# The first layer job's clipped-square activation: last step moved from VectorE to GpSimd

## The reference, cut to what matters

```python
scores = q @ k.T / 8                       # 4 batches, 8 heads, 576 rows, 64 wide
attn   = softmax(scores where they are among the row's 32 largest)
x      = attn @ v                          # laid out as 2304 tokens x 512
h      = x @ w_in                          # layer 1, 2048 wide
g      = where(h >= 1, h, where(h <= -1, 0, (h + 1)**2 / 4))
x      = g @ w_out
h      = maximum(x @ w_in2, 0)             # layer 2
out    = (h * h) @ w_out2
```

## Time and profile before

| | |
|---|---|
| Median of 3 runs | 1271.18 us (1269.45 to 1271.53) |
| The profiled execution | 1268.48 us, its span 1266.7 us |
| PE busy in the span | 1189.1 us, 94% |
| DVE / ACT / POOL busy | 846.9 / 799.9 / 748.4 us |
| The stretch of job 0's activations on DVE | 127.7 to 219.8 us |

### The profile page before, as it was taken

The page is one execution under the profiler, slowest core; times in us unless marked ns, Lnnn a source line. Parts: engine busy times, 40 slices in busy tenths (PEclk is TensorE's granted clock), DMA queues, the critical chain, the costliest instruction groups (busy, mean ns, idle before and its releaser), DMA issues.

```text
span 1266.7 us, 24472 instructions
## 1 busy us (share of the span) xinstructions
PE 1189.1 (94%) x8760; PEld 1130.0 (89%) x8760; DVE 846.9 (67%) x1894; ACT 799.9 (63%) x1797; POOL 748.4 (59%) x620
## 2 busy tenths in 40 slices
PE   3777888999999999999999999999999999999998
PEld 2667888988889999999999999999999999999997
DVE  7898999899798799989899987878740111110000
ACT  6887666767666667676666766566654565654443
POOL 4778678777888676777857675755652222222222
PEclk9756999999999999999999999999999999999999
DMA  7798456675879953154348841456439400780000
GB/s 259 266 360 326 183 205 241 225 280 193 307 279 362 388 206 105 64 170 141 126 143 287 299 150 45 126 177 201 124 118 369 172 34 1 292 306 18 18 17 17
DMA packets 96264, 240.65 MB, mean 190 GB/s; under 512 B 7824, under 2 KB 47760, under 8 KB 83856
## 3 DMA queue, kind: packets, MB, share of 16 engines
q1 hardware_dynamic: 96144, 239.09, 52.9%
HBM read 167.23 MB, written 71.83 MB: 189 GB/s over the span
## 4 chain that ended last, share of the span: by engine, by line
PE 71%; ACT 9%; DVE 8%; POOL 5%; issue 3%; DMA 3%; SPq 0%; ACTq 0%; POOLq 0%
PE h_ps L600 21%; PE y_ps L621 15%; PE y_ps L615 11%; PE pv_ps L559 6%; PE score_ps L600 6%; DVE top L903 4%; PE tr_ps L532 4%; PE score_ps L497 3%; DVE rest L905 3%; ACT prob L718 2%; POOL s_sb L1085 2%; POOL prob L1090 1%; POOL kq_lo L1068 1%; ACT s_sb L695 1%; PE pv_ps L571 1%
## 5 line engine op out<-in xcount | busy, mean ns | idle before, releaser
L1103 POOL TENSOR_TENSOR g_lo<-g_sb,g_hi 128x256 fp32r<-128x256 f32 x288 | 217.5, 755 | 415.4 <-ACT g_hi L813 226.9
L600 PE MATMUL h_ps<-xt_hi,w_in 128*128 128x256 f32 x1880 | 391.0, 291 | 3.5 <-DVE xt_lo L951 1.7
L600 PEld LDWEIGHTS h_ps<-xt_hi,w_in 128*128 128x128 f32 x1880 | 309.3, 191 | 6.4 <-ACT r_sb L795 2.3
L903 DVE MAX8 top<-rest 128x8 f32<-128x576 f32 x432 | 304.4, 745 | 0.4
L600 PE MATMUL h_ps<-xt_lo,w_in 128*128 128x256 f32 x940 | 266.1, 283 | 0.0
L1085 POOL TENSOR_SCALAR s_sb<-s_sb,top 128x576 f32<-128x576 f32 x126 | 223.9, 1777 | 44.2 <-DVE top L903 44.1
L615 PE MATMUL y_ps<-g_hi,w_out 128*128 128x256 f32 x1152 | 231.8, 284 | 0.4 <-POOL g_lo L1103 0.3
L905 DVE MATCH_REPLACE8 rest<-top,rest 128x576 f32<-128x576 f32 x288 | 211.4, 740 | 0.0
L621 PE MATMUL y_ps<-w_out,g_hi 128*128 128x512 f32 x576 | 203.2, 394 | 0.3 <-ACT ys L779 0.3
L615 PEld LDWEIGHTS y_ps<-g_hi,w_out 128*128 128x128 f32 x1152 | 189.6, 192 | 1.9 <-POOL g_lo L1103 0.5
L1090 POOL TENSOR_TENSOR prob<-s_sb,prob 128x576 f32<-128x576 f32 x128 | 182.3, 1427 | 9.2
(11 more groups left out here) (87 smaller groups left out, 2022.4 us busy)
## 6 DMA issues: line engine op xcount, KB each, us to landing
w_in<-w_scratch SPq DMA_DIRECT2D x32, 1024.0 KB, 6.8
w_out<-w_scratch SPq DMA_DIRECT2D x32, 1024.0 KB, 8.1
ks<-kq_scratch SPq DMA_DIRECT2D x47, 576.0 KB, 5.5
qs<-kq_scratch SPq DMA_DIRECT2D x156, 128.0 KB, 4.2
w_scratch<-w_in SPq DMA_DIRECT2D x16, 1024.0 KB, 7.5
w_scratch<-w_out SPq DMA_DIRECT2D x16, 1024.0 KB, 8.0
v_sb<-in_vv_dram SPq DMA_DIRECT2D x48, 325.0 KB, 5.1
stage<-in_w_dram SPq DMA_DIRECT2D x24, 512.0 KB, 5.4
```

Source lines behind the costliest of these rows:

```text
L600: last = pe.matmul(h_bank(k), wi[:, f // 2, w, m, cols], x[:, m, :], start=(m == 0 and n == 0), stop=(m == KT - 1 and n == 2))
L903: dve.max(best, src[:, :]).then_inc(rank_step, 1)
L1103: pool.tensor_tensor(g_lo[k % 2][:, :], g_sb[k % 2][:, :], g_hi[k % 2][:, :].bitcast(F32), ALU.subtract).then_inc(g_lo_done, 1)
```

## The change

For the 16 steps of job 0 (k < 16) ACT computes a third relu, r = relu(r - 2), in place, after the square; POOL adds it to the square, g = u + r, and raises `g_done`; DVE does nothing for these steps. For h >= 1 the square is 1 and the relu is h - 1; below that the relu is 0. All other steps of layer 1 stay on DVE, which now also waits for the `g_done` of the step before. The bias -2 comes from a new one-column tile, set by POOL at the start. In a slot POOL's order becomes mask(n-1, 0), sum(q), mask(n-1, 1), lo(q), sum(q+1), lo(q+1).

```diff
+def summed_by_pool(k):
+    return k < FT
...
+        minus_two = sb("minus_two", [P, 1])
...
+                if k == 0:
+                    act.wait_ge(constants_set, 2)
...
-                act.activation(u[:, :], u[:, :], ACT.Square, bias=1.0, scale=-0.5).then_inc(squared, 1)
+                if not summed_by_pool(k):
+                    act.activation(u[:, :], u[:, :], ACT.Square, bias=1.0, scale=-0.5).then_inc(squared, 1)
+                    return
+                act.activation(u[:, :], u[:, :], ACT.Square, bias=1.0, scale=-0.5)
+                act.activation(r[:, :], r[:, :], ACT.Relu, bias=minus_two[:, 0:1]).then_inc(squared, 1)
...
-                if JOBS[k // FT][0] == 1:
+                if JOBS[k // FT][0] == 1 and not summed_by_pool(k):
                     dve.wait_ge(squared, CURVED[k] + 1)
+                    dve.wait_ge(g_done, CURVED[k])
...
+            def sum_at(q):
+                k = UP_AT.get(q)
+                if k is not None and summed_by_pool(k):
+                    pool.wait_ge(squared, CURVED[k] + 1)
+                    pool.tensor_tensor(g_sb[k % 2][:, :], g_sb[k % 2][:, :], r_sb[k % 2][:, :],
+                                       ALU.add).then_inc(g_done, 1)
...
                 lo_at(q - 1)
+                sum_at(q)
                 if before:
                     mask(n - 1, 1)
                 lo_at(q)
+                sum_at(q + 1)
                 lo_at(q + 1)
...
+            pool.memset(minus_two[:, :], -2.0)
             pool.memset(ident[:, :], 0.0).then_inc(constants_set, 1)
```

## The result

The changed kernel takes 1274.85 us in the median of 20 runs (1270.75 to 1280.86), the kernel before 1269.17 us in as many (1265.48 to 1272.54). The ratio is 1.0046, with a 95% interval of 1.0035 to 1.0057: 5.8 us slower (4.4 to 7.2). The profiled execution took 1271.36 us, its span 1269.6.

What follows compares the result with a forecast made beforehand. Slots 11 to 17 were taken as bound by a ring of all engines, later work by PE. Slot terms summed to 5.05 us slower: 1273.5 us against the profiled execution, 1276 for the median, range 1271 to 1280.5.

Steps and rivals of the forecast that it cites:

- The ring: Slots 11 to 17: PE, ACT and POOL wait for each other in a cycle; DVE alone does not set the pace.
- the loop of 11.65 us: Cycle without DVE: first relu, square and new relu, POOL's add, second mask, transposes, PE, next first relu; 11.65 us.
- Slot 10: One extra relu on ACT ahead of copy_shared, for which PE's times_v waits; +0.42 us.
- Slot 11: First relu to next first relu: 11.68 us before, 11.65 with the change; -0.03 us.
- Slot 14: First relu to next first relu: 11.27 us before, 11.65 with the change; +0.38 us.
- Pairs: Slots 12-13 and 15-16: two relus +0.84, add between POOL's masks +0.70, contention -0.17; +1.37 us each.
- the 0.17 given back: POOL's second mask compare no longer meets a DVE activation, so it shortens by about 0.17 us.
- Last stretch: Slot 17 until PE's transpose in slot 18: +0.84 for relus, +0.70 for the add, no contention returned; +1.54 us.
- The relu: ACT's added activation with a bias tile costs 0.42 us per step, bounds 0.33 and 0.51.
- The add: POOL's added 128x256 TENSOR_TENSOR costs 0.70 us per step, bounds 0.62 and 0.76.
- Passing the whole loss to the end: After slot 18's transpose PE has no room, so all 5.05 us reach the end; 2.5 if half is absorbed.
- The rival on DVE: DVE sets the pace, so relieving it is faster: ceiling 15.3 us, a third of it gives 1266; chance 0.10.

Runs made afterwards that it cites:

- the second profiles: One more profiled execution each of the unmodified change and of the kernel before; stretch from slot 12 82.57 us and 78.23 us.
- the kernel with kq on DVE: The change with the kq subtraction of slots 12, 15 and 17 moved from POOL to the end of DVE's slot; 1.0061 of the kernel before.
- the kernel without the sum: The change without ACT's third relu and POOL's add, DVE's job 0 work still gone, the square alone used as g; 0.9986 of the kernel before.
- the load-only kernel: The kernel before plus same-size POOL adds on a spare tile at the change's places, waiting for no other engine; 1.0013 of the kernel before.
- add behind both masks: The change with POOL's add of each slot's first step moved behind the second mask; 1.0131 of the kernel before.
- second step only: The change applied only to each slot's second step, the first step staying on DVE; 1.0018 of the kernel before.
- second step and kq on DVE: The change for each slot's second step only, plus the kq subtraction of slots 12, 15 and 17 on DVE; 1.0009 of the kernel before.

## Why the prediction was right

Forecast 1276.0 (1271 to 1280.5), measured 1274.85; forecast +5.05 us, measured +5.8 (4.4 to 7.2), and +5.05 in the first two profiles from job 0's first relu on. The ring was right: which engines wait for which, the loop of 11.65 us, and what each added instruction costs in its queue. Two things in the close numbers are luck. The sum meets 5.05 to the hundredth because its errors cancel (-0.1 in each pair, +0.3 in the last stretch), and the second profiles say 4.4. And the forecast of 1276 stood on a median of three runs, 1271.18; over 20 runs the kernel before has 1269.17, 2.0 lower, and 1269.17 + 5.05 would have been 1274.2.

- Slot 10: +0.42 forecast, 6.68 instead of 6.28 us: +0.40.
- Slot 11: the loop of 11.65 us, measured 11.62. Slot 14: 11.66. The loop without DVE is confirmed to 0.03 us, with POOL's idle 1.80 us inside it, and again by slots 13 and 16 of the kernel with kq on DVE (11.68 and 11.65).
- Pairs: +1.37 forecast, +1.25 and +1.26 measured (25.41 against 24.16 and 24.15). The add cost 0.71 and two relus 0.80; less the 0.17 given back that is 1.34, so 0.1 us of the difference is not accounted for.
- Last stretch: +1.54 forecast; measured 225.34 - 205.27 = 20.07 against 18.26: +1.81. The term is short by 0.3: in slot 18 the add waited 0.38 us for ACT, which I had taken as covered there. It also said that slot 17 had no contention to give back, but before, the second compare there took 1.95 us (slots 12 and 14: 1.97 and 1.96), after 1.73. What that gave back is not shown.
- The relu: the distance from the new activation to the next is 169.85 - 169.45 = 0.40 us, against 0.42. (The Trainium skill, "ScalarE: Activation LUTs", section "What ACT_TABLE_LOAD costs", gives 93 ns for a bias read from a tile; here the instruction took 0.49 us beside 0.42 without one, 0.07 more, so the trace has it a little smaller.)
- The add: 0.73 us, 0.71 to the next instruction, against 0.70.
- Passing the whole loss to the end was right for the change: the tail is 1044.3 us after and 1044.5 before, and 1044.8 and 1046.5 in the second profiles. It does not hold for every version: two stages shorter by 2 and 5 us gave no shorter time.
- The rival on DVE is refuted by the kernel without the sum: -1.8 us (at most 2.9), where it gave 5 us for a third of its ceiling and the expectation 10. The rival of hidden additions is refuted by the load-only kernel, 2.5 us longer in the stretch, and "no change" by the measured difference of 4.4 to 7.2 us.
- The rival of a falling clock did not strike the change's two profiles, but did strike three relatives of it (add behind both masks, second step only, second step and kq on DVE). I had given it together with another mechanism 0.09; how often it strikes the executions without a profile is open.

## What to carry to other kernels

Before you take work off the busiest engine, look at what releases it and whom it releases: in a ring of engines with orders written out by hand, 9.4 us of work on an engine that was 94% busy were worth 1.8 us when they were taken away for nothing. Price a moved instruction by what stands behind it in its new queue, and ask above all what new wait it puts in front of work that did not need it. Look also at what it will run beside: in three versions here a DVE subtraction that was moved met a POOL instruction, which grew by 1.2 to 1.6 us. And confirm a gain in a stage by the time of many runs: two versions here were shorter in their stage by 2 and 5 us and no faster.

## What the runs showed of the hardware

- A POOL TENSOR_TENSOR of 128x256 that met a DVE TENSOR_TENSOR with both inputs in SBUF took 2.02 us instead of 0.73, and the DVE one its ordinary 1.41. A POOL TENSOR_SCALAR of 128x576 that met the same DVE subtraction took 3.29 us instead of 1.72. (This is the exclusion that the Trainium skill describes in "SBUF — State Buffer", section "Who interferes with whom"; the trace agrees.)
- The granted clock can fall in the middle of dense work. In the kernel with the second step only, after a 4 us window in which PE was busy 2.29 us the next shows 0.60, and after one with 2.33 us 0.50; eight transposes at 218.22 us took 1.91 us there, against 1.04 at a clock of 1.00. Thin windows alone don't settle it: in the kernel with kq on DVE PE is busy 1.29 us in one window, and the clock stays at 1.00.

```profile
184.00:188.00 4.00, 1.29 (x10) 0.92 (x9) 3.87 (x6) 3.88 (x8) 3.92 (x4) 1.00 0.04 17
188.00:192.00 4.00, 4.00 (x38) 4.00 (x36) 2.68 (x7) 0.77 (x3) 3.33 (x4) 1.00 1.02 376
```

- Ahead of slot 12 the same program varies by 1.9 us (before) and 1.8 us (the change) between its two profiles. In all four the clock lies between its two levels there: from 44 to 124 us their 4 us windows show 0.50 to 0.93.
